# A chunked linear recurrence with routed layers: the order of VectorE's work over four chunks, and the engine that masks the grams

## The chip, the cores and the metric

One NeuronCore of a Trainium2 chip runs the whole program. The metric is the device time of one execution in microseconds (us), lower is better. Engines are named as in the profile: PE is TensorE, DVE VectorE, ACT ScalarE, POOL GpSimd, SP the engine that only issues transfers.

## What is computed

Inputs r, k, v, w, a, b are (4 batches, 8 heads, 768 steps, 40 channels), all float32. Each of the 32 pairs of batch and head runs a recurrence over a 40x40 state:

```python
for t in range(768):
    y[:, :, t] = np.einsum('bhd,bhde->bhe', rt, state)
    Sa = np.einsum('bhde,bhe->bhd', state, at)
    state = state * wt[:, :, None, :] - np.einsum('bhd,bhe->bhde', Sa, bt)
    state = state + np.einsum('bhd,bhe->bhde', vt, kt)
```

y goes, as 3072 tokens of 320 values, through a layer of 8 experts (the best two of noisy gates, 320 to 1024 to 320, relu) and a dense layer (320 to 2048 to 320, leaky relu). The change touches the recurrence alone.

## The kernel before

Four stages follow one another: `stage_a` is the recurrence, `stage_r` the routing, `stage_e` the experts, `stage_m` the dense layer. Only `stage_a` matters here. It lays the recurrence out in 24 chunks of 32 steps, indexed `k`; four chunks make a group `s` of 128 steps (`s = k // 4`, place in the group `c = k % 4`, `NS_` = 6 groups, `NK` = 24 chunks). The state (`S0T`) is handed from chunk to chunk. For each group there are products that don't need the state, made ahead of time:

- `suffix(s)` (DVE) turns the loaded decays `P` into running products, `prefix(s)` (DVE) does so for `U`. `make_A`, `make_B`, `make_K` (POOL) multiply the loaded `AT` with `U` and `BT`, `KT` with `P`.
- The grams: `lb(s, c)` (PE, from `AT` and `BT`) gives the coupling of the steps inside a chunk; ACT copies it to `LbS`, SP writes it to DRAM (`out_half`), reads it back by lanes (`to_lanes`, tile `Lt`), and DVE inverts it there by substitution: `inverse(s)` is a generator of 63 steps, first the clearing of `Tl` (after a wait for `Lt` and for the write of the last `Tl`), then for t = 1 to 31 a product `prod` of t x t elements (L331) and a reduction (L335). The result goes to DRAM and back as blocks (`from_lanes`, `to_blocks`, tile `TT`, 16 transfers), for `solve` on PE.
- `lk(s, c)` (from `KT` and `AT`) goes to `LkT`, `gv(k)` to `GvT`, `gp(k)` to `Gpb`. ACT copies each out of PSUM, and each is then multiplied in place by a triangular mask `pos_m` or `neg_m`: `mask_lk`, `mask_gv`, `mask_gp`.

PE runs a hand-written order: in chunk k it does `first(k)` (L532), a gram of a later group, `turn_S(k)` (L596), `grow_K`, `solve(k)` (L606), `read_S(k-1)`, `add_B(k-1)` (L648, needs the masked `Gpb` of k-1), `turn_P`, `gv`, `grow_B`, tokens or rows, a second gram, `add_K(k-1)` (L658, needs the masked `GvT` of k-1), `gp(k)` (L665), and `lkv(k+1)` (L542, needs the masked `LkT`). `turn_S(k)` writes the banks in which the outputs of chunk k-2 lie, so it waits until DVE has read them: `pe.wait_ge(q["v_y"], k - 1)`, that is, until `y_out(k-2)` (L355) is done. `first(k)` at c = 0 waits for `decay(s-1)` (L344), which scales the state by `Wend`.

SP's queue is in order too. At c = 2 and 3 it issues `out_half(s+2, c-2)`, which waits for ACT's copies of the grams `lb`; at c = 3 there follow, in this order:

```python
                if c >= 2 and s + 2 < NS_:
                    out_half(s + 2, c - 2)
                if c == 3 and s + 1 < NS_:
                    from_lanes(s + 1)
                    if s + 2 < NS_:
                        to_lanes(s + 2)
                    to_blocks(s + 1)
                    if s + 3 < NS_:
                        suffix_in(s + 3)
```

`from_lanes(s+1)` waits for the end of `inverse(s+1)`; `suffix_in(s+3)` is the load of `P`. At the next c = 0 the loads of `AT`, `BT`, `KT` follow, and at c = 1 that of `U`, which waits for `v_y` of 4s, the last output of the group before. `zeros` are loads into `xsort` that nothing here waits for; ACT issues `RV` and `Vd` for chunk k+2 at the end of each chunk.

DVE takes, in each chunk, `y_out(k-2)` and then a number of steps of `inverse(s+1)`: 14, 12, 18 and the 19 that are left, with `suffix(s+2)` after eight steps at c = 0 and `prefix(s+2)` after eleven at c = 1; `decay` comes at the start of the next group.

Of the kernel before, what the change touches and what calls it, by code (L numbers as in the profile page):

```python
# [21 lines left out]
ALU = mybir.AluOpType  # L22
# [5 lines left out]
CH = 32  # L28
NS_ = S // SC
NK = S // CH  # L30
# [12 lines left out]
def stage_a(nc, st, wE, wR, aE, bE, kE, rvE, vG, cst, wgh, zer, lscr, tscr, xrow, xsort):  # L43
    ctx = ExitStack()
    with ctx:
# [3 lines left out]
        def sem(name):  # L49
# [4 lines left out]
        pos_m = sb("pos_m", [128, CH])  # L54
        neg_m = sb("neg_m", [128, 128])
# [12 lines left out]
        LkT = sb("LkT", [128, 2, 4, 2, 4, CH])  # L68
# [16 lines left out]
                 "l_lw l_lane l_tw l_t0 l_t1 l_t2 l_t3 l_zf l_x0 l_x1 "  # L85
                 "z_v z_g e_A e_B e_K v_P v_U v_end v_dve v_inv v_y v_S "
                 "o_S o_X o_y p_X p_Gv p_G p_Str p_P p_tok p_rows p_PT p_S p_y p_Gp "
                 "a_X a_gv a_G a_S0 a_Pn a_tok a_row a_PT a_S a_Gp g_lk g_gv g_gp").split()
        q = {n: sem(n) for n in names}
        block = ctx.enter_context(nc.Block())  # L90
        TOKS = {0: (0,), 1: (), 2: (1, 2), 3: (3,)}
# [1 line left out]
        def slot(k):  # L93
            return k // 4, k % 4
# [11 lines left out]
        def round_lk(s, c):  # L106
            return 4 + c if s == 0 else before(4 * (s - 1) + c // 2) + c % 2
# [113 lines left out]
        def _(pool):  # L221
# [20 lines left out]
                    i = tt(t, t, P[:, :, CH * c:CH * c + CH].rearrange("p (b h) t -> p h b t", b=NB), ALU.mult)  # L242
                i.then_inc(q["e_K"], 1)

            def mask_lk(s, c):
                pool.wait_ge(q["a_G"], round_lk(s, c) + 1)
                t = LkT[:, s % 2, c, :, :, :].rearrange("p h g t -> p (h g) t")
                tt(t, t, pos_m[:, :].rearrange("p (o t) -> p o t", o=1).to_broadcast([128, 8, CH]), ALU.mult).then_inc(q["g_lk"], 1)

            def mask_gv(k):  # L250
                pool.wait_ge(q["a_gv"], k + 1)
                t = GvT[:, k % 2, :, :, :].rearrange("p h b t -> p (h b) t")
                tt(t, t, pos_m[:, :].rearrange("p (o t) -> p o t", o=1).to_broadcast([128, 8, CH]), ALU.mult).then_inc(q["g_gv"], 1)

            def mask_gp(k):
                pool.wait_ge(q["a_Gp"], k + 1)
                t = Gpb[:, :, :, :].rearrange("p b h m -> p (b h) m")
                tt(t, t, neg_m[:, :].rearrange("p (o t) -> p o t", o=1).to_broadcast([128, 8, 128]), ALU.mult).then_inc(q["g_gp"], 1)

            make_A(0, 0)  # L260
            make_A(0, 1)
            make_K(0)
            pool.wait_ge(q["l_c"], 80)
            for c in range(4):
                mask_lk(0, c)
            for j in range(2):
                make_A(1, j)
                make_B(1, j)
            make_K(1)
            for k in range(NK):  # L270
                s, c = slot(k)
                mask_gv(k)
                if c < 2 and s + 1 < NS_:
                    mask_lk(s + 1, 2 * c)
                    mask_lk(s + 1, 2 * c + 1)
                if c == 1 and s + 2 < NS_:
                    for j in range(2):
                        make_A(s + 2, j)
                        make_B(s + 2, j)
                if c == 2 and s + 2 < NS_:  # L280
                    make_K(s + 2)
                mask_gp(k)

        @block.vector
        def _(dve):
# [63 lines left out]
            def y_out(k):  # L349
                s, c = slot(k)  # L350
                dve.wait_ge(q["p_y"], k + 1)
                if k and c == 0:
# [3 lines left out]
                                        ps[0:EP, 2:4, 0:256].rearrange("p i (g t) -> p i g t", t=CH),  # L356
                                        U[:, s % 3, :, t].rearrange("p (i g) t -> p i g t", i=2), ALU.mult).then_inc(q["v_y"], 1)

            nc.vector.memset(ps[:, :, :], 0.0).then_inc(q["z_v"], 1)
            nc.vector.memset(start[:, :], 0.0).then_inc(q["z_v"], 1)  # L360
            dve.wait_ge(q["z_v"], 2)
# [14 lines left out]
            prefix(1)  # L376
            for _ in T:
                pass
            steps = {0: 14, 1: 12, 2: 18, 3: 64}
            for k in range(NK + 2):  # L380
                s, c = slot(k)
                if k < NK and c == 0:
                    T = inverse(s + 1) if s + 1 < NS_ else iter(())
                    if k:
                        decay(s - 1)
                if k >= 2:
                    y_out(k - 2)
                if k >= NK:
                    continue
                for i in range(steps[c]):  # L390
                    if c == 0 and i == 8 and s + 2 < NS_:
                        suffix(s + 2)
                    if c == 1 and i == 11 and s + 2 < NS_:
                        prefix(s + 2)
                    next(T, None)

        @block.scalar
        def _(act):
# [121 lines left out]
        def _(pe):  # L520
# [15 lines left out]
            def lkv(k):  # L536
                s, c = slot(k)
                pe.wait_ge(q[f"l_g{k % 2}"], 16 * (k // 2 + 1))
                pe.wait_ge(q["g_lk"], 4 * s + c + 1)
                for p in range(2):  # L540
                    for h in range(4):
                        m = mm(ps[Z_[h], 4 + p, 0:NB * D], LkT[:, s % 2, c, p, h, :], Vd[:, k % 2, p, h, :],  # L542
                               start=True, stop=False, skip_group_check=True)
                m.then_inc(q["o_X"], 1)
# [146 lines left out]
            for k in range(NK + 1):  # L691
# [29 lines left out]
                if k:  # L721
                    if k < NK:
                        pe.wait_ge(q["a_S0"], k + 1)
                    else:
                        pe.wait_ge(q["v_y"], k - 1)
                    read_S(k - 1, 0)
                    pe.wait_ge(q["g_gp"], k)
                    add_B(k - 1)
                if k < NK:
                    pe.wait_ge(q["a_PT"], k + 1)  # L730
# [15 lines left out]
                if k:  # L746
                    pe.wait_ge(q["o_y"], 4 * k - 3)
                    read_S(k - 1, 1)
                    pe.wait_ge(q["g_gv"], k)
                    pe.wait_ge(q["o_y"], 4 * k - 1)  # L750
                    add_K(k - 1, 0)
                if k < NK:
# [691 lines left out]
```

## Time and profile before

| | us |
|---|---|
| median of 3 runs | 1638.34 (1636.05 to 1650.76) |
| the profiled execution's own time | 1636.78 |
| its span | 1635.0 |
| busy in the span: PE, DVE, ACT, POOL | 1341.4, 909.5, 655.1, 304.8 |

The time of an execution is that of its span and 1.8 us around it. The span's first 642 us are the recurrence; in rows of the profile, a time such as 275.39 is counted from the start of the span, "idle before" is how long the engine had nothing running, and the name behind the arrow is what ended that. Busy shares over the whole span say little about the recurrence, since the later stages have other limits.

### The profile page before, as it was taken

What the parts mean: (1) busy time and instruction counts of PE and PEld (TensorE: products, weight loads), DVE (VectorE), ACT (ScalarE), POOL (GpSimd) and SP (SyncE); (2) the same over time, 40 slices, a digit from 0 to 9 for tenths busy, and PEclk for the clock granted to TensorE, in tenths of its full rate; (3) what the DMA queues carried; (4) which work ended last, traced back from release to release, by engine and by line L of the source; (5) the groups of instructions that cost most, each with busy time, mean ns of one, the idle gap of its engine ahead of it and who ended that gap; (6) DMA issues with size and microseconds to landing.
All of it is one profiled execution on the core that took longest, in us unless ns stands there. A gap on an engine that the chain in (4) does not pass through costs nothing. (4 is left out here: it accounts for less than half of the span.)

```text
span 1635.0 us, 40604 instructions
## 1 busy us (share of the span) xinstructions
PE 1341.4 (82%) x16814; PEld 1217.7 (74%) x16814; DVE 909.5 (56%) x1553; ACT 655.1 (40%) x1451; POOL 304.8 (19%) x253
## 2 busy tenths in 40 slices
PE   3549698888979796004999999999993999999998
PEld 3437586666868585004999999999993889889887
DVE  4857557492663401504777777778772453554533
ACT  3314334343434122203666666666661333333332
POOL 3316132241411110570000000000003210110000
PEclk9957767686687665556999999999997999999999
DMA  6753554748352222735676676676661110110000
GB/s 153 176 112 100 126 157 119 202 119 193 113 145 81 76 71 64 266 120 172 216 259 216 218 255 218 219 253 218 222 214 53 53 32 17 49 38 10 16 17 16
DMA packets 149248, 219.58 MB, mean 134 GB/s; under 512 B 61210, under 2 KB 120474, under 8 KB 145722
## 3 DMA queue, kind: packets, MB, share of 16 engines
q1 hardware_dynamic: 132143, 163.84, 34.4%
q10 hardware_dynamic: 9891, 27.97, 5.8%
q0 software_dynamic: 7088, 25.89, 4.8%
q8 instruction: 103, 1.69, 0.4%
q14 instruction: 23, 0.19, 0.0%
HBM read 185.49 MB, written 42.34 MB: 139 GB/s over the span
## 5 line engine op out<-in xcount | busy, mean ns | idle before, releaser
L1232 DVE TENSOR_TENSOR gf<-psM,low 128x512 f32<-128x512 f32 x96 | 66.4, 692 | 179.3 <-ACT low L1270 179.3
L331 DVE TENSOR_TENSOR prod<-Tl,Lt 128x1 f32<-128x1 f32 (+30 forms) x186 | 142.9, 768 | 38.0 <-DMA Lt<-lscr 31.9
L1075 PE MATMUL psE<-w2h,hh 128*128 128x320 f32 x496 | 155.9, 314 | 0.0
L1270 ACT ACTIVATE low<-psM 128x512 f32<-128x512 f32 x96 | 57.5, 599 | 242.6 <-PE psM L1328 242.6
L1077 PE MATMUL psE<-w2h,hl 128*128 128x320 f32 x496 | 153.5, 309 | 0.0
L1076 PE MATMUL psE<-w2l,hh 128*128 128x320 f32 x496 | 153.4, 309 | 0.0
L1060 PE MATMUL psE<-xh,w1h 128*128 128x256 f32 x496 | 141.6, 285 | 5.6 <-DVE w1l L965 5.6
L1061 PE MATMUL psE<-xl,w1h 128*128 128x256 f32 x496 | 141.5, 285 | 0.0
L1062 PE MATMUL psE<-xh,w1l 128*128 128x256 f32 x496 | 141.5, 285 | 0.0
L965 DVE TENSOR_TENSOR w2l<-w2t,w2h 128x320 fp32r<-128x320 f32 x248 | 122.1, 492 | 10.8 <-ACT w2h L960 10.8
L1307 PE MATMUL psM<-woh,gh 128*128 128x320 f32 x384 | 120.1, 313 | 2.9 <-DVE gl L965 2.5
L1132 DVE SCALAR_TENSOR_TENSOR hl<-psE,hh 128x256 fp32r<-128x256 f32 x248 | 105.4, 425 | 27.6 <-ACT hh L1101 4.3
L1309 PE MATMUL psM<-woh,gl 128*128 128x320 f32 x384 | 118.8, 309 | 0.0
L1308 PE MATMUL psM<-wol,gh 128*128 128x320 f32 x384 | 118.7, 309 | 0.0
L1101 ACT ACTIVATE hh<-psE 128x256 fp32r<-128x256 f32 x248 | 95.0, 383 | 55.2 <-PE psE L1064 52.9
L960 ACT ACTIVATE w2h<-w2t 128x320 fp32r<-128x320 f32 x248 | 114.8, 463 | 0.0
L1147 POOL DMA_DIRECT2D ysort<-ys x31 | 22.2, 717 | 483.8 <-DVE ys L1139 483.8
L965 DVE TENSOR_TENSOR w1l<-w1t,w1h 128x1024 fp32r<-128x1024 f32 (+1 forms) x93 | 108.1, 1218 | 2.1
L1042 PE MATMUL psE<-ident,xs 128*128 128x128 f32 x186 | 26.1, 278 | 92.2 <-DMA w1t<-in_w_dram 92.2
L1060 PEld LDWEIGHTS psE<-xh,w1h 128*128 128x128 f32 x496 | 96.3, 194 | 6.0 <-issue 6.0
L335 DVE TENSOR_REDUCE Tl<-prod 128x1 f32<-128x1 f32 (+30 forms) x186 | 93.7, 504 | 5.9
L355 DVE TENSOR_TENSOR xT<-psA,U 104x512 f32<-104x512 f32 x24 | 16.5, 689 | 144.2 <-PE psA L658 144.2
(170 smaller groups left out, 3378.9 us busy)
## 6 DMA issues: line engine op xcount, KB each, us to landing
w2t<-in_w_dram SPq DMA_DIRECT2D x31, 1280.0 KB, 6.2
w1t<-in_w_dram SPq DMA_DIRECT2D x31, 1024.0 KB, 8.1
w1t<-in_w_dram SPq DMA_DIRECT2D x62, 256.0 KB, 8.8
Vd<-in_vG_dram ACTq DMA_DIRECT2D x22, 640.0 KB, 6.2
xs<-xsort SPq DMA_DIRECT2D x31, 320.0 KB, 5.7
ysort<-ys POOLq DMA_DIRECT2D x31, 320.0 KB, 4.3
xsort<-in_zer_dram SPq DMA_DIRECT2D x15, 640.0 KB, 8.3
RV<-in_rvE_dram ACTq DMA_DIRECT2D x22, 416.0 KB
```

The source lines that it names most:

```text
L331: mark(nc.vector.tensor_tensor(prod[:, 0:t, 0:t], Tl[:, 0:t, CH - t:CH], Lt[:, t:t + 1, CH - t:CH].to_broadcast([128, t, t]), ALU.mult))
L960: return nc.scalar.activation(hi, src, ACT.Copy)
L965: return nc.vector.tensor_tensor(lo, src, hi.bitcast(F32), ALU.subtract)
L1060: mm(o, w1h[:, j, fs], xh[:, p, j, :], start=(j == 0), stop=False)
L1061: mm(o, w1h[:, j, fs], xl[:, p, j, :], start=False, stop=False)
L1062: mm(o, w1l[:, j, fs], xh[:, p, j, :], start=False, stop=False)
L1075: mm(o, hh[:, f, sl], w2h[:, f, :], start=(f == 0), stop=False)
L1076: mm(o, hh[:, f, sl], w2l[:, f, :], start=False, stop=False)
L1077: m = mm(o, hl[:, f, sl], w2h[:, f, :], start=False, stop=(f == NF - 1))
L1307: mm(o, gh[:, f % 4, sl], woh[:, f, :], start=(f == 0), stop=False)
L1308: mm(o, gh[:, f % 4, sl], wol[:, f, :], start=False, stop=False)
L1309: m = mm(o, gl[:, f % 4, sl], woh[:, f, :], start=False, stop=(f == NF - 1))
```

## The change

On POOL `mask_lk` stays for group 0 alone, the other masks go, and `make_B`, `make_K`, `make_A` get a new order. On DVE the masks are added, each waiting for ACT's copy, and the steps of the inversion, `suffix`, `prefix` and `decay` get new places: 10 + 17 steps at c = 0 behind `suffix`, 10 + 8 at c = 1, 6 + 6 at c = 2, 6 at c = 3, with `decay(s)` at the end of c = 3. PE's order is as it was; only the names of what it waits for change. SP and ACT are untouched.

```diff
--- before.py
+++ after.py
@@ -85,7 +85,7 @@
                  "l_lw l_lane l_tw l_t0 l_t1 l_t2 l_t3 l_zf l_x0 l_x1 "
                  "z_v z_g e_A e_B e_K v_P v_U v_end v_dve v_inv v_y v_S "
                  "o_S o_X o_y p_X p_Gv p_G p_Str p_P p_tok p_rows p_PT p_S p_y p_Gp "
-                 "a_X a_gv a_G a_S0 a_Pn a_tok a_row a_PT a_S a_Gp g_lk g_gv g_gp").split()
+                 "a_X a_gv a_G a_S0 a_Pn a_tok a_row a_PT a_S a_Gp g_lk v_lk v_gv v_gp").split()
         q = {n: sem(n) for n in names}
         block = ctx.enter_context(nc.Block())
         TOKS = {0: (0,), 1: (), 2: (1, 2), 3: (3,)}
@@ -242,44 +242,30 @@
                     i = tt(t, t, P[:, :, CH * c:CH * c + CH].rearrange("p (b h) t -> p h b t", b=NB), ALU.mult)
                 i.then_inc(q["e_K"], 1)
 
-            def mask_lk(s, c):
-                pool.wait_ge(q["a_G"], round_lk(s, c) + 1)
-                t = LkT[:, s % 2, c, :, :, :].rearrange("p h g t -> p (h g) t")
+            def mask_lk(c):
+                pool.wait_ge(q["a_G"], round_lk(0, c) + 1)
+                t = LkT[:, 0, c, :, :, :].rearrange("p h g t -> p (h g) t")
                 tt(t, t, pos_m[:, :].rearrange("p (o t) -> p o t", o=1).to_broadcast([128, 8, CH]), ALU.mult).then_inc(q["g_lk"], 1)
-
-            def mask_gv(k):
-                pool.wait_ge(q["a_gv"], k + 1)
-                t = GvT[:, k % 2, :, :, :].rearrange("p h b t -> p (h b) t")
-                tt(t, t, pos_m[:, :].rearrange("p (o t) -> p o t", o=1).to_broadcast([128, 8, CH]), ALU.mult).then_inc(q["g_gv"], 1)
-
-            def mask_gp(k):
-                pool.wait_ge(q["a_Gp"], k + 1)
-                t = Gpb[:, :, :, :].rearrange("p b h m -> p (b h) m")
-                tt(t, t, neg_m[:, :].rearrange("p (o t) -> p o t", o=1).to_broadcast([128, 8, 128]), ALU.mult).then_inc(q["g_gp"], 1)
 
             make_A(0, 0)
             make_A(0, 1)
             make_K(0)
             pool.wait_ge(q["l_c"], 80)
             for c in range(4):
-                mask_lk(0, c)
+                mask_lk(c)
             for j in range(2):
                 make_A(1, j)
                 make_B(1, j)
             make_K(1)
             for k in range(NK):
                 s, c = slot(k)
-                mask_gv(k)
-                if c < 2 and s + 1 < NS_:
-                    mask_lk(s + 1, 2 * c)
-                    mask_lk(s + 1, 2 * c + 1)
+                if c == 0 and s + 2 < NS_:
+                    make_B(s + 2, 0)
+                    make_B(s + 2, 1)
                 if c == 1 and s + 2 < NS_:
-                    for j in range(2):
-                        make_A(s + 2, j)
-                        make_B(s + 2, j)
-                if c == 2 and s + 2 < NS_:
                     make_K(s + 2)
-                mask_gp(k)
+                    make_A(s + 2, 0)
+                    make_A(s + 2, 1)
 
         @block.vector
         def _(dve):
@@ -356,6 +342,24 @@
                                         ps[0:EP, 2:4, 0:256].rearrange("p i (g t) -> p i g t", t=CH),
                                         U[:, s % 3, :, t].rearrange("p (i g) t -> p i g t", i=2), ALU.mult).then_inc(q["v_y"], 1)
 
+            def tiled(m, n):
+                return m.rearrange("p (o t) -> p o t", o=1).to_broadcast([128, 8, n])
+
+            def mask_lk(s, c):
+                dve.wait_ge(q["a_G"], round_lk(s, c) + 1)
+                t = LkT[:, s % 2, c, :, :, :].rearrange("p h g t -> p (h g) t")
+                nc.vector.tensor_tensor(t, t, tiled(pos_m[:, :], CH), ALU.mult).then_inc(q["v_lk"], 1)
+
+            def mask_gv(k):
+                dve.wait_ge(q["a_gv"], k + 1)
+                t = GvT[:, k % 2, :, :, :].rearrange("p h b t -> p (h b) t")
+                nc.vector.tensor_tensor(t, t, tiled(pos_m[:, :], CH), ALU.mult).then_inc(q["v_gv"], 1)
+
+            def mask_gp(k):
+                dve.wait_ge(q["a_Gp"], k + 1)
+                t = Gpb[:, :, :, :].rearrange("p b h m -> p (b h) m")
+                nc.vector.tensor_tensor(t, t, tiled(neg_m[:, :], 128), ALU.mult).then_inc(q["v_gp"], 1)
+
             nc.vector.memset(ps[:, :, :], 0.0).then_inc(q["z_v"], 1)
             nc.vector.memset(start[:, :], 0.0).then_inc(q["z_v"], 1)
             dve.wait_ge(q["z_v"], 2)
@@ -376,23 +380,51 @@
             prefix(1)
             for _ in T:
                 pass
-            steps = {0: 14, 1: 12, 2: 18, 3: 64}
+            dve.wait_ge(q["l_c"], 80)
             for k in range(NK + 2):
                 s, c = slot(k)
+
+                def invert(n):
+                    for _ in range(n):
+                        next(T, None)
+
                 if k < NK and c == 0:
                     T = inverse(s + 1) if s + 1 < NS_ else iter(())
-                    if k:
-                        decay(s - 1)
                 if k >= 2:
                     y_out(k - 2)
+                if 1 <= k <= NK:
+                    mask_gp(k - 1)
                 if k >= NK:
                     continue
-                for i in range(steps[c]):
-                    if c == 0 and i == 8 and s + 2 < NS_:
+                if c == 0:
+                    if s + 2 < NS_:
                         suffix(s + 2)
-                    if c == 1 and i == 11 and s + 2 < NS_:
+                    invert(10)
+                    mask_gv(k)
+                    if s + 1 < NS_:
+                        mask_lk(s + 1, 0)
+                    invert(17)
+                    if s + 1 < NS_:
+                        mask_lk(s + 1, 1)
+                elif c == 1:
+                    invert(10)
+                    mask_gv(k)
+                    if s + 1 < NS_:
+                        mask_lk(s + 1, 2)
+                    if s + 2 < NS_:
                         prefix(s + 2)
-                    next(T, None)
+                    invert(8)
+                    if s + 1 < NS_:
+                        mask_lk(s + 1, 3)
+                elif c == 2:
+                    invert(6)
+                    mask_gv(k)
+                    invert(6)
+                else:
+                    invert(6)
+                    mask_gv(k)
+                    if s + 1 < NS_:
+                        decay(s)
 
         @block.scalar
         def _(act):
@@ -536,7 +568,7 @@
             def lkv(k):
                 s, c = slot(k)
                 pe.wait_ge(q[f"l_g{k % 2}"], 16 * (k // 2 + 1))
-                pe.wait_ge(q["g_lk"], 4 * s + c + 1)
+                pe.wait_ge(q["v_lk" if s else "g_lk"], 4 * (s - 1 if s else 0) + c + 1)
                 for p in range(2):
                     for h in range(4):
                         m = mm(ps[Z_[h], 4 + p, 0:NB * D], LkT[:, s % 2, c, p, h, :], Vd[:, k % 2, p, h, :],
@@ -724,7 +756,7 @@
                     else:
                         pe.wait_ge(q["v_y"], k - 1)
                     read_S(k - 1, 0)
-                    pe.wait_ge(q["g_gp"], k)
+                    pe.wait_ge(q["v_gp"], k)
                     add_B(k - 1)
                 if k < NK:
                     pe.wait_ge(q["a_PT"], k + 1)
@@ -746,7 +778,7 @@
                 if k:
                     pe.wait_ge(q["o_y"], 4 * k - 3)
                     read_S(k - 1, 1)
-                    pe.wait_ge(q["g_gv"], k)
+                    pe.wait_ge(q["v_gv"], k)
                     pe.wait_ge(q["o_y"], 4 * k - 1)
                     add_K(k - 1, 0)
                 if k < NK:
```

## Rows read from the trace of the kernel before

**Rows 1.** Windows by chunk (4, 5, 16): length, busy by engine, PEclk, DMA share, GB/s.

```profile
179.60:199.20 19.60, 18.74 (x459) 14.66 (x461) 2.65 (x10) 8.28 (x20) 2.68 (x4) 0.76 0.68 130
199.20:235.40 36.20, 28.59 (x492) 24.92 (x492) 16.79 (x36) 9.81 (x28) 9.30 (x7) 0.59 0.69 180
...
466.10:485.70 19.60, 18.72 (x456) 14.62 (x457) 4.84 (x19) 8.28 (x20) 2.54 (x4) 0.76 0.72 160
```

**Rows 2.** Waits, 0 to 650 us: who <- whom, us in total, times, longest.

```profile
PE psA L606 <- DMA TT<-tscr: 23.0, 2, 20.0
PE psA L532 <- DVE S0T L344: 22.7, 5, 5.6
...
PE psA L596 <- DVE xT L355: 5.6, 2, 3.2
```

**Rows 3.** PE's timeline, chunks 7 to 11: start, duration, engine, line, [idle before <-releaser].

```profile
253.28 0.77 PE L532 MATMUL psA<-S0T,AT 40*32 40x40 f32 x64 [0.18 <-PE psA L542]
...
275.39 0.94 PE L532 MATMUL psA<-S0T,AT 40*32 40x40 f32 x64 [4.57 <-DVE S0T L344]
...
303.39 1.65 PE L596 MATMUL psA<-ident,S0T 104*128 104x104 f32 x8 [3.16 <-DVE xT L355]
...
328.92 0.93 PE L532 MATMUL psA<-S0T,AT 40*32 40x40 f32 x64 [0.18 <-PE psA L542]
...
346.10 0.77 PE L532 MATMUL psA<-S0T,AT 40*32 40x40 f32 x64 [0.18 <-PE psA L542]
```

**Rows 4.** Timeline of SP and DVE from the end of chunk 7.

```profile
266.81 0.35 SPq L147 DMA_DIRECT2D lscr<-LbS  x1
...
274.64 0.32 SPq L161 DMA_DIRECT2D tscr<-Tl  x1
...
291.06 0.58 SPq L132 DMA_DIRECT2D xsort<-in_zer_dram  x1
...
294.79 0.06 DVE L299 MEMSET start<- 104x4 f32 x1 [11.66 <-DMA P<-in_wR_dram]
...
302.65 0.68 DVE L355 TENSOR_TENSOR xT<-psA,U 104x512 f32<-104x512 f32 x1
```

**Rows 5.** Instructions by line, 0 to 600 us.

```profile
L242 POOL TENSOR_TENSOR KT<-KT,P 104x512 f32<-104x512 f32 x24 | 31.5, 1345 | 0.2 <-DMA KT<-in_kE_dram 0.2
...
L367 DVE TENSOR_TENSOR BT<-BT,P 104x1024 f32<-104x1024 f32 x2 | 2.3, 1210 | 0.0
```

**Rows 6.** Waits of SP's queue, 0 to 640 us.

```profile
SPq L155 <- DMA lscr<-LbS: 3.2, 1, 3.2
```

**Rows 7.** DVE's small steps, t = 1 and t = 7.

```profile
472.58 0.16 DVE L331 TENSOR_TENSOR prod<-Tl,Lt 128x1 f32<-128x1 f32 x1 [2.75 <-DMA Lt<-lscr]
...
475.07 0.21 DVE L331 TENSOR_TENSOR prod<-Tl,Lt 128x49 f32<-128x49 f32 x1
```

**Rows 8.** DVE beside POOL at chunk 17.

```profile
485.30 2.34 POOL L258 TENSOR_TENSOR Gpb<-Gpb,neg_m 128x1024 f32<-128x1024 f32 x1 [1.56 <-ACT Gpb L402]
485.50 2.23 DVE L331 TENSOR_TENSOR prod<-Tl,Lt 128x64 f32<-128x64 f32 x1
...
490.48 0.34 DVE L331 TENSOR_TENSOR prod<-Tl,Lt 128x169 f32<-128x169 f32 x1
```

**Rows 9.** The transfer that SP issued at 291.06: size, us to landing.

```profile
xsort<-in_zer_dram SPq DMA_DIRECT2D x1, 640.0 KB, 23.0
```

**Rows 10.** DVE and POOL at chunk 2.

```profile
139.74 2.19 POOL L235 TENSOR_TENSOR BT<-BT,P 104x1024 f32<-104x1024 f32 x1
...
140.69 3.60 DVE L331 TENSOR_TENSOR prod<-Tl,Lt 128x196 f32<-128x196 f32 x1
...
141.88 2.20 POOL L229 TENSOR_TENSOR AT<-AT,U 104x1024 f32<-104x1024 f32 x1
```

**Rows 11.** Chunks 0 to 1.

```profile
114.66 0.06 DVE L299 MEMSET start<- 104x4 f32 x1 [10.56 <-DMA P<-in_wR_dram]
...
127.11 1.07 PE L648 MATMUL psA<-Gpb,Bk 128*40 128x128 f32 x16
```

## The prediction

> **What bounds the kernel now.** I read the page's row of busy shares by slice, then windows by chunk, then who waited for whom, then the timelines around the longest waits. Only the first 642 us of the span can change. There PE is the engine that work passes through: it is busy 18.7 of the 19.6 us of chunk 4, but only 28.6 of the 36.2 us of chunk 5, at a mean granted clock of 0.76 and 0.59 [rows 1], so part of its time is waiting and part is the half clock around the waits. The waits by name are three [rows 2]: for the scaled state at the start of a group (22.7 us in five times), for `y_out` of the last chunk of the old group at `turn_S` of chunk 4s+1 (5.6 us, two times), and for the inverse's blocks (23.0 us, of which 20.0 at the very start and 3.0 in group 5). Behind them stands a loop over three queues. I measure a group from the start of its predecessor's chunk c = 3, here chunk 7 at 253.28 [rows 3]:
>
> - SP passes `out_half` at 266.81, which is 13.5 us in, when ACT has copied the last gram; the inverse, which is DVE's long tail of 19 steps, ends just before SP's next issue at 274.64; `P` lands at 294.79, 20.15 us after that (21.8 and 22.1 us in the two other groups of this kind) [rows 4].
> - DVE, which stood idle 11.66 us for `P`, does `suffix`, six small steps and `y_out` by 303.33, 8.5 us later (7.0 and 6.9 in the two other groups, where no POOL instruction fell on the scans) [rows 4]. PE's `turn_S(9)` starts at 303.39 after a wait of 3.16 us [rows 3].
> - From there PE takes 25.5 us to the start of chunk 10 and 17.2 more to chunk 11 [rows 3], where the loop closes.
>
> So `turn_S(9)` starts 50.1 us behind the start of chunk 7 (49.3 and 49.2 in the two other groups), and this number, not the sum of DVE's work, decides the recurrence's pace.
>
> **The change: what it gives.** `decay(s)` follows in chunk c = 3 behind six steps and `mask_gv`. Six steps are at most six instructions of 1.21 us, the duration of a product of 1024 elements [rows 5], 7.3 us; with `y_out` (0.68 [rows 4]) and `mask_gp` (1.2, by the same row of 1024 elements) DVE is through after 9.2 us of a chunk in which PE has 16 us of work. The waits at `first` go: 22.7 us. The inverse then ends at most 9.2 us into chunk 7, not 21.4. But SP can't use that: `out_half(s+2, 1)` stands ahead of `from_lanes` in its queue and passes 13.5 us in [rows 4]. Of 12 us that the inverse gains, 7.9 reach the queue. Of these, 2.5 go again: `to_lanes` waits for the write of `LbS`, which had 7.8 us of lead and now is issued right ahead; the bounds are 0 and the 3.2 us that such a wait once took [rows 6]. A further 2.0 go since ACT's loads `RV` and `Vd` (1.08 MB by their shapes) leave at the end of chunk 7 and now meet the small block transfers; bounds 0 and 6.7, all of it at 160 GB/s [rows 1]. With 21.3 as the mean from the issue to the landing, `P` lands 13.5 + 2.5 + 21.3 + 2.0 = 39.3 us into the count (34 to 45), where it was 41.5: a gain of 2.2.
>
> The masks leave POOL, where nothing but DVE felt them; PE waited once for one, 1.3 us at the end, which goes.
>
> **What it costs.** `y_out(4s-1)` now stands behind all of c = 0: `suffix`, 27 steps and three masks, and PE's `turn_S(4s+1)` is who waits. From the landing of `P`:
>
> - what was there before: 7.0;
> - the clearing of `Tl`, 1.0 (1024 elements, estimate by the 1.21 of [rows 5]), and seven first steps that used to be done while `P` was on its way: 13 steps from t = 1 to the product of t = 7 take 2.7 us [rows 7], so 1.4;
> - 13 more steps, to t = 13: from the product of t = 8 to that of t = 13 are 5.3 us, of which 2.0 are blocking (next item) [rows 8]; with the two reductions at the ends 3.9;
> - three masks of 256 elements: a quarter of 1.21, 1.0 in all.
>
> That is 14.3 us. To it comes the blocking. A product of 64 elements beside POOL's mask took 2.23 us and ended with it [rows 8], where one of 169 took 0.34. In the new order POOL starts `make_B` twice and `make_K` right behind `suffix`, as soon as `BT` and `KT` are there. These follow `P` in SP's queue. The last transfer of that series lands at 291.06 + 23.0 = 314.06 [rows 4, 9]; `AT`, `BT`, `KT` (832 KB each by shape) and its own 640 KB moved in the 17.9 us since 296.2, when the `zeros` ahead of them was in by the same view, so `BT` is there some 11 us and `KT` some 16 us behind `P` (an estimate by bytes). Two `make_B` of 2.2 us [rows 10] then fall on the small steps, each holding up one product: 3.5. Of four `make_K` instructions of 1.35 us [rows 5] the last one or two products and the last mask meet up to three: between 0 and 3.6, and I take 1.2, since most of the steps are done by then. Sum 19.0 us (14.3 to 21.5), against 7.0 to 8.5.
>
> How long one product is held has a rule beside it. In chunk 2 a product of 196 elements started at 140.69 while POOL's `BT` ran until 141.93, and it ended 3.60 us later, after the next POOL instruction too [rows 10]. The Trainium skill, "SBUF — State Buffer", section "SBUF: two separate sides", says that the port pair VectorE and GpSimd share is a lock, held for a whole instruction by whichever starts first. By that rule a waiting product would lose one POOL instruction at most; by the row it can lose two. By the row, both `make_B` may fall on one product, and the steps behind it start some 0.5 us later than by the rule, 19.5 in place of 19.0.
>
> So `turn_S` of c = 1 starts 39.3 + 19.0 = 58.3 us into the count: 8.2, 9.0 and 9.1 us later than before in groups 1, 2 and 3 taken together, 26.3. PE's wait there becomes some 18 us (its own work reaches `turn_S` 16 + 22.7 us in), and takes the place of both old waits. It adds nothing elsewhere: `prefix` waits for `U`, issued with `y_out(4s-1)`, but chunk c = 1 is the long one, 25.5 us behind `turn_S` [rows 3]. The masks' own waits cover themselves: `mask_gv` waits for a copy in mid-chunk, and behind it at c = 2 stand six steps of under 1.2 us each, which fit ahead of the chunk's end.
>
> In group 0 there is no `y_out` to wait for, but `mask_gp(0)` stands behind the same list. `P` is there at 114.66 [rows 11], no `zeros` are ahead of `BT`, so all of `make_K` falls on the steps: 114.66 + 14.3 - 0.7 + 3.5 + 3.0 + 1.2 = 136.0, while `add_B(0)` started at 127.11 [rows 11]. PE waits 8.8 us (2.3 to 10). `y_out(0)` at chunk 2 then comes late by 2.7 more (0 to 5), behind `prefix` and 18 steps. Together 11.5.
>
> After the last `suffix`, in groups 4 and 5, the change only gives: the wait at chunk 16 (5.4 of the 22.7), at chunk 20 (1.7), that for the blocks (3.0), the mask (1.3), and the half clock behind the two waits. Chunk 16 ran at 0.76 [rows 1]; a quarter of its 19.6 us is lost to the clock and I give back 3.0, and 2.0 in chunk 20. Sum 16.4. The four other waits at `first` are inside the counts above. For a shorter c = 1, with the loads behind it and fewer gaps in PE's fetching, I take off 1.0 each, 3.0.
>
> **Sum.** 26.3 + 11.5 - 16.4 - 3.0 = +18.4 us. The profiled execution took 1636.8 us; it becomes 1655.2. It lies 1.6 below the median shown, so in terms of the median it is about 1656.
>
> **Rivals.** *The wait moves and costs nothing.* POOL's instructions find DVE idle, or `KT` lands late, and the small steps run unblocked: 14.3 in place of 19.0, and group 0 loses 3 in place of 11.5. Then 12.2 + 3 - 16.4 - 3.0 = -4, 1633 to 1645 around it. For it: the product of t = 13 and its neighbours are short, 0.3 us [rows 8], and rarely meet anything. Against: [rows 8] shows that even 64 elements wait.
>
> *Faster: the chain from the inverse to `P` shortens.* Its 16 block transfers ran beside the first chunk's loads; started 8 us sooner they may take less, with neither the 2.5 nor the 2.0 paid. The point from which it decides is `turn_S` at 49.5 us into the count. At 13.5 + 18 + 14.3 = 45.8 each group gains 3.7, in all -11 + 3 - 16.4 - 3.0 = -27, about 1610. For it: the gain at `first` is certain. Against: it needs all three terms at their low ends.
>
> *Slower still.* All terms at their high ends, 45 + 21.5 = 66.5 us: 17 more a group, 1680. Chunk 5 was at 0.59 of the full clock already [rows 1], so little is left to lose there.
>
> **How the numbers follow.** The sum as worked out (1646 to 1672) 0.5; the unblocked case 0.28; the faster one 0.13; the heavier one 0.09. A measurement of this kernel tells changes of over 1%, 16.4 us, from none, so the bounds are 1622 and 1655. Above 1655 lie half of the first case, part of the space between, and the last: 0.45. Below 1622 lies the faster case with an edge of the second: 0.15. Within 0.40. The range 1618 to 1672 leaves out the faster case and the heavier one.
>
> **What would show it.** Right: PE's wait at L532 for S0T gone; a wait of PE at L596 for DVE xT of 12 to 20 us in each of groups 1 to 3; at L648 for DVE Gpb of some 9 us in chunk 1; SP's `tscr` issue right behind the `lscr` issue, 13 to 14 us into c = 3; DVE idle for `P` over 20 us; products at t = 8 to 13 of over 1.3 us. Wrong: L596 waits of under 8 us, small steps without blocking, or `P` landing less than 34 us into the count.

## The result and the profile after

The changed kernel takes 1660.4 us (median of 4 runs, 1658.4 to 1666.8), the kernel before 1641.6 (4 runs). The medians lie 18.8 us apart; the ratio is 1.013, with a 95% interval of 1.009 to 1.017, so the loss is 14 to 28 us. The forecast was 1656. The execution that was profiled took 1666.8 us, the longest of the four, so its rows show some 6 us more than the median has, while the profile of the kernel before (1636.8) is 5 us below its own median. The two profiles lie 30.0 us apart, and some 11 us of that is the spread of executions.

The waits by name, 0 to 680 us (who <- whom, us in total, times, longest). In the changed file L564 is `first`, L628 `turn_S`, L638 `solve`, L680 `add_B`, L285 the start of `suffix`, L341 `y_out`:

```profile
DVE start L285 <- DMA P<-in_wR_dram: 87.9, 5, 24.3
...
PE psA L628 <- DVE xT L341: 34.5, 4, 11.4
...
PE psA L638 <- DMA TT<-tscr: 33.0, 5, 19.5
...
PE psA L680 <- DVE Gpb L361: 9.0, 2, 8.6
```

Beside [rows 2]: the wait at `first` for the scaled state (22.7 us) has left the list. The one at `turn_S` for `y_out` has grown from 5.6 to 34.5, the one at `solve` for blocks from 23.0 to 33.0, and `add_B`, which waited 1.3 us for a mask once, now waits 8.6 us for one in chunk 1.

The same stretch as in [rows 3, 4], chunks 7 to 10, on PE, then SP and DVE:

```profile
273.67 0.77 PE L564 MATMUL psA<-S0T,AT 40*32 40x40 f32 x64 [0.18 <-PE psA L574]
...
291.50 0.93 PE L564 MATMUL psA<-S0T,AT 40*32 40x40 f32 x64 [0.18 <-PE psA L574]
...
311.64 0.63 PE L564 MATMUL psA<-S0T,AT 40*32 40x40 f32 x49 [0.18 <-PE psA L574]
...
328.87 1.65 PE L628 MATMUL psA<-ident,S0T 104*128 104x104 f32 x8 [9.39 <-DVE xT L341]
...
355.57 0.93 PE L564 MATMUL psA<-S0T,AT 40*32 40x40 f32 x64 [0.18 <-PE psA L574]
```

```profile
280.20 1.16 DVE L321 TENSOR_REDUCE Tl<-prod 128x31 f32<-128x961 f32 x1
...
287.31 0.35 SPq L147 DMA_DIRECT2D lscr<-LbS  x1
287.84 0.32 SPq L161 DMA_DIRECT2D tscr<-Tl  x1
...
306.26 1.42 SPq L127 DMA_DIRECT2D P<-in_wR_dram  x1
...
314.29 0.06 DVE L285 MEMSET start<- 104x4 f32 x1 [22.30 <-DMA P<-in_wR_dram]
...
328.13 0.69 DVE L341 TENSOR_TENSOR xT<-psA,U 104x512 f32<-104x512 f32 x1
```

Read from the start of chunk 7 (273.67): SP passes the gram's write 13.6 us in and issues the inverse right behind it, although DVE had ended it at 281.36, 6.5 us before that issue (5.9, 11.9 and 7.2 us in chunks 3, 11 and 15); `P` lands 40.6 us in; `y_out` ends after 55.2 us, and `turn_S(9)` starts with it. Before, those were 13.5, 41.5 and 50.1. Chunk 8 starts without a wait at its head, 17.8 us in, where it was 22.1.

Windows of chunks 4, 5 and 16, columns as in [rows 1]:

```profile
187.30:213.30 26.00, 21.78 (x458) 16.98 (x460) 1.65 (x3) 8.29 (x20) 0.00 (x0) 0.70 0.78 153
213.30:255.30 42.00, 26.78 (x492) 23.20 (x493) 38.47 (x69) 9.81 (x28) 15.07 (x8) 0.58 0.50 135
495.80:521.20 25.40, 18.02 (x456) 14.05 (x457) 10.17 (x34) 8.29 (x20) 0.00 (x0) 0.83 0.83 178
```

DVE is nearly idle in chunk 4 (1.65 us of 26.0) and full in chunk 5 (38.5 of 42.0): its work was not spread. Chunk 16 grew from 19.6 to 25.4 us; PE waits 6.4 us in it for blocks, at `solve`.

DVE and POOL behind `P`'s landing in group 1, at 212.11 (start, duration):

```profile
222.50 4.31 POOL L235 TENSOR_TENSOR BT<-BT,P 104x1024 f32<-104x1024 f32 x2 [71.25 <-DMA BT<-in_bE_dram]
222.54 2.23 DVE L317 TENSOR_TENSOR prod<-Tl,Lt 128x81 f32<-128x81 f32 x1
...
225.08 1.84 DVE L317 TENSOR_TENSOR prod<-Tl,Lt 128x100 f32<-128x100 f32 x1
...
227.96 5.98 POOL L242 TENSOR_TENSOR KT<-KT,P 104x512 f32<-104x512 f32 x4 [1.16 <-DMA KT<-in_kE_dram]
```

`BT` is there 10.4 us behind `P`, `KT` 15.9 us (estimated: 11 and 16). Each `make_B` held up one product, t = 9 by 2.0 and t = 10 by 1.6 us. In group 2 SP had issued one more of the `zeros` ahead of these loads, and `BT` came only 16.3 us behind `P`, after `y_out`: no step was held there. In group 3 it came 12.2 us behind `P`.

### The profile page after: what moved, and what is told of

It is laid out like the page before. It is cut to its first block and busy times, and to the rows that moved or that the text cites. A ratio compares the mean times of both kernels' runs of the same rounds, so it can differ in the third digit from the quotient of the medians.

```text
span 1665.1 us, 40604 instructions
## 1 busy us (share of the span) xinstructions
PE 1349.9 (81%) x16814; PEld 1221.4 (73%) x16814; DVE 940.4 (56%) x1621; ACT 655.8 (39%) x1451; POOL 213.6 (13%) x185
## 3 DMA queue, kind: packets, MB, share of 16 engines
q8 instruction: 103, 1.69, 0.4%
## 5 line engine op out<-in xcount | busy, mean ns | idle before, releaser
L317 DVE TENSOR_TENSOR prod<-Tl,Lt 128x1 f32<-128x1 f32 (+30 forms) x186 | 130.2, 700 | 29.4 <-DMA Lt<-lscr 23.6
L1164 DVE SCALAR_TENSOR_TENSOR hl<-psE,hh 128x256 fp32r<-128x256 f32 x248 | 105.4, 425 | 27.6 <-ACT hh L1133 4.4
L1094 PEld LDWEIGHTS psE<-xh,w1l 128*128 128x128 f32 x496 | 96.2, 194 | 0.0
L1093 PEld LDWEIGHTS psE<-xl,w1h 128*128 128x128 f32 x496 | 96.1, 194 | 0.0
```

The lines of the kernel that those rows point to most:

```text
L317: mark(nc.vector.tensor_tensor(prod[:, 0:t, 0:t], Tl[:, 0:t, CH - t:CH], Lt[:, t:t + 1, CH - t:CH].to_broadcast([128, t, t]), ALU.mult))
L1093: mm(o, w1h[:, j, fs], xl[:, p, j, :], start=False, stop=False)
L1094: mm(o, w1l[:, j, fs], xh[:, p, j, :], start=False, stop=False)
```

## The experiments

Each kernel is compared with the kernel before, run on the same chip in turn, whose median was 1642.8, 1642.2 and 1640.5 us in the three rounds; "ratio" is its time over that. The changed kernel's 1.013 comes from a round of its own, with four executions on each side.

**One part at a time.** The masks alone, the same three helpers defined on DVE (`mask_lk` of group 0 stays on POOL):

```diff
             for k in range(NK):
                 s, c = slot(k)
-                mask_gv(k)
-                if c < 2 and s + 1 < NS_:
-                    mask_lk(s + 1, 2 * c)
-                    mask_lk(s + 1, 2 * c + 1)
...
-                mask_gp(k)
...
                 if k >= 2:
                     y_out(k - 2)
+                if 1 <= k <= NK:
+                    mask_gp(k - 1)
...
                     next(T, None)
+                mask_gv(k)
+                if c < 2 and s + 1 < NS_:
+                    mask_lk(s + 1, 2 * c)
+                    mask_lk(s + 1, 2 * c + 1)
```

> The order of before on DVE (14, 12, 18 and 19 steps, decay at the start of the next group) and on POOL for make_A, make_B, make_K; only the masks are moved to DVE, mask_gp behind y_out, mask_gv and mask_lk at the end of a chunk's steps. Theory (the time went into y_out of the last chunk of a group, which stands behind all of c = 0): the masks add 1.6 us a chunk to DVE, of which some 2 us stand ahead of decay in c = 3, and take away blocking by POOL of 1 to 2 us there; 0 to 3 us a group, 1638 to 1652 us, and the wait at turn_S of c = 1 stays under 5 us. Rival (the masks themselves cost it, by DVE's work and its waits for ACT): most of the 20 us, 1655 or more.

1641.3 us, ratio 0.999 (0.996 to 1.002). The waits of its profile:

```profile
PE psA L620 <- DMA TT<-tscr: 24.2, 6, 18.4
...
PE psA L546 <- DVE S0T L329: 10.5, 4, 4.6
PE psA L610 <- DVE xT L340: 10.3, 3, 5.4
...
PE psA L576 <- POOL BT L235: 4.3, 1, 4.3
```

The masks cost nothing; the wait for the scaled state (L546) even halves, while the one at `turn_S` (L610) doubles. The rival that blames the masks by themselves is out.

The order alone:

```diff
+                if c == 1 and s + 2 < NS_:
+                    make_K(s + 2)
                 mask_gv(k)
...
                 if c == 1 and s + 2 < NS_:
-                    for j in range(2):
-                        make_A(s + 2, j)
-                        make_B(s + 2, j)
-                if c == 2 and s + 2 < NS_:
-                    make_K(s + 2)
+                    make_A(s + 2, 0)
+                    make_A(s + 2, 1)
                 mask_gp(k)
+                if c == 0 and s + 2 < NS_:
+                    make_B(s + 2, 0)
+                    make_B(s + 2, 1)
...
-                    if k:
-                        decay(s - 1)
...
-                for i in range(steps[c]):
-                    if c == 0 and i == 8 and s + 2 < NS_:
-                        suffix(s + 2)
-                    if c == 1 and i == 11 and s + 2 < NS_:
+                if c == 0 and s + 2 < NS_:
+                    suffix(s + 2)
+                for i in range((27, 18, 12, 6)[c]):
+                    if c == 1 and i == 10 and s + 2 < NS_:
                         prefix(s + 2)
                     next(T, None)
+                if c == 3 and s + 1 < NS_:
+                    decay(s)
```

> The new order of steps, suffix, prefix and decay on DVE, but all masks stay on POOL, with mask_gp of c = 0 ahead of make_B and the masks of c = 1 behind make_K. Theory: turn_S of c = 1 waits as in the changed kernel, less 1 us for the masks that are gone, 8 to 11 us in groups 1 to 3; the wait of add_B(0) for the mask (8.6 us) goes; 1646 to 1655 us. Rival (the masks cost it): the waits go with the masks, 1620 to 1640 us.

1671.1 us, ratio 1.016 (1.011 to 1.021). The order alone (on DVE and on POOL) loses at least as much as the whole change. My range ended 16 us too low, since I had thought that it would be a little cheaper than the whole change. Its waits at `turn_S` are 42.3 us in four, 12.6 at most. From `P` to `turn_S` it takes 20.3, 17.6 and 19.1 us in groups 1 to 3, where the changed kernel takes 19.3, 14.6 and 17.7. In groups 2 and 3 POOL's `mask_gp` falls beside DVE's scans of `P`, which take 6.64 us in place of 4.61. In group 2:

```profile
316.80 2.35 POOL L258 TENSOR_TENSOR Gpb<-Gpb,neg_m 128x1024 f32<-128x1024 f32 x1 [2.24 <-ACT Gpb L403]
316.87 0.06 DVE L301 MEMSET start<- 104x4 f32 x1 [23.64 <-DMA P<-in_wR_dram]
316.96 6.64 DVE L306 TENSOR_TENSOR_SCAN P<-P,start 104x516 f32<-104x516 f32 x4
```

So here the masks on POOL do cost something that they don't cost on DVE. Whether that is the whole of the difference was not tried.

**The blocking.** The changed kernel with `make_A`, `make_B` in turn behind `prefix` and `make_K` at c = 2:

```diff
-                if c == 0 and s + 2 < NS_:
-                    make_B(s + 2, 0)
-                    make_B(s + 2, 1)
                 if c == 1 and s + 2 < NS_:
-                    make_K(s + 2)
-                    make_A(s + 2, 0)
-                    make_A(s + 2, 1)
+                    for j in range(2):
+                        make_A(s + 2, j)
+                        make_B(s + 2, j)
+                if c == 2 and s + 2 < NS_:
+                    make_K(s + 2)
```

> The changed kernel with make_B and make_K of POOL back in their old places (A, B, A, B behind prefix, K at c = 2), so that no POOL instruction falls on the small steps of c = 0. Theory with blocking: from P's landing to y_out it takes 14.3 us in place of 14.6 to 19.3, the wait of add_B(0) falls from 8.6 to 2.5 us; PE has to wait a little for BT at c = 2; 1643 to 1652 us. Rival (blocking doesn't matter, the steps are hidden): 1658 to 1663 us.

1653.4 us, ratio 1.007 (1.003 to 1.011). From `P`'s landing to the end of `y_out`, in group 1:

```profile
208.65 0.06 DVE L284 MEMSET start<- 104x4 f32 x1 [25.06 <-DMA P<-in_wR_dram]
...
222.50 0.69 DVE L340 TENSOR_TENSOR xT<-psA,U 104x512 f32<-104x512 f32 x1
```

14.5 us where the sum for unblocked steps was 14.3, and 19.3 in the changed kernel. It takes 14.5 us in groups 2 and 3 too. The wait of `add_B(0)` is 3.5 in place of 8.6 us, and one of 2.6 us for `BT` is new in chunk 2. So the blocking is real and is gone. What it is worth in the whole is less sure: 7.0 us of 18.8 by the medians, 0.6 of 1.3 points by the ratios, whose intervals overlap. The waits at `turn_S` fell only from 34.5 to 31.8 us in total, as PE came to them earlier.

**`y_out` out of the way of `P`.** The changed kernel with `suffix` in c = 1:

```diff
                 if c == 0:
-                    if s + 2 < NS_:
-                        suffix(s + 2)
                     invert(10)
...
                 elif c == 1:
+                    if s + 2 < NS_:
+                        suffix(s + 2)
                     invert(10)
```

> The changed kernel with suffix(s+2) moved from the start of c = 0 to c = 1, behind y_out and mask_gp, so that y_out of the old group's last chunk waits for no load. Theory: the waits of turn_S in c = 1 (9.4 to 11.4 us, three) and of add_B(0) (8.6 us) go; the loop then closes over the load of U and make_A at c = 2, where PE waits up to 7 us a group; 1610 to 1635 us. Rival (the masks cost it): no gain, 1655 us or more.

1642.7 us, ratio 1.001 (0.998 to 1.004). The loss is gone, as the theory says and the rival (no gain, 1655 us or more) does not; but the 1610 to 1635 I had expected was not reached. Waits:

```profile
PE psA L638 <- DMA TT<-tscr: 28.2, 5, 18.8
...
PE psA L564 <- issue: 9.4, 3, 4.3
PE psA L671 <- issue: 7.4, 4, 3.4
PE psA L628 <- DVE xT L341: 7.4, 2, 3.8
```

At `turn_S` 7.4 us are left of 34.5. The wait for `make_A` at c = 2 that I had expected did not come. What stays is the blocks at `solve` (28.2 with the 18.8 of the very start, so 9.4 where the kernel before had 3.0), and what came forward is "issue", time in which PE waited for nothing that the profile shows. PE's sum of "issue" over 76 to 642 us is 29.2 us in the kernel before, 28.2 in the changed one and 37.4 here.

**SP's queue.** The next four kernels change where SP issues. The loads of `P` ahead of `out_half`:

```diff
+                if c == 3 and s + 3 < NS_:
+                    suffix_in(s + 3)
                 if c == 0 and s + 2 < NS_:
...
                     to_blocks(s + 1)
-                    if s + 3 < NS_:
-                        suffix_in(s + 3)
```

> The changed kernel, but SP issues the load of P for suffix(s+3) at the start of c = 3, ahead of out_half, instead of behind the block transfers. Theory (what costs is the wait for P, 22 to 24 us of idle VectorE, with y_out behind it): P is there when c = 0 begins, the waits of turn_S in c = 1 of groups 1 to 3 (9.4 to 11.4 us) fall under 3 us, and what remains late is the blocks at solve in c = 0, 2 to 6 us a group; group 0 is unchanged; 1625 to 1645 us. Rival (the order on VectorE is simply too long for the chunk, whatever the load does): the waits stay over 7 us, 1655 or more.

1650.2 us, ratio 1.006 (1.004 to 1.009). The waits of `turn_S(4s+1)` are gone in all three groups, and DVE no longer waits for `P` there. What stays is group 0 (9.1 us at `add_B`), blocks at 1.9 to 3.0 us a group, and 36.5 us of "issue". So the waits behind `P` are gone, and half of the loss stayed; 5 us slower than expected.

The blocks ahead:

```diff
+                if c == 3 and s + 1 < NS_:
+                    from_lanes(s + 1)
+                    to_blocks(s + 1)
                 if c >= 2 and s + 2 < NS_:
                     out_half(s + 2, c - 2)
                 if c == 3 and s + 1 < NS_:
-                    from_lanes(s + 1)
                     if s + 2 < NS_:
                         to_lanes(s + 2)
-                    to_blocks(s + 1)
```

> The changed kernel, but SP issues from_lanes and to_blocks at c = 3 ahead of out_half(s+2, 1), to_lanes behind it. Theory: the inverse that ends 9 us into c = 3 now reaches SP; the waits of solve for blocks at c = 0 (2.8, 1.6, 2.7, 6.4 us) go. In groups 1 to 3 nothing comes of it unless P lands earlier too, since turn_S waits later in the same stretch; P stands behind to_lanes, whose gate is as before, but the 16 block transfers (8 us) are no longer ahead of it, so P lands up to 8 us earlier: 1625 to 1650 us. Rival (the blocks' transfers cost the same wherever they stand, P does not come earlier): 1650 to 1660 us.

1647.8 us, ratio 1.004 (1.000 to 1.007). Two lines of its waits:

```profile
PE psA L629 <- DVE xT L342: 31.4, 4, 12.1
...
PE psA L639 <- DMA TT<-tscr: 19.7, 1, 19.7
```

Only the very first wait for blocks is left, the other four (2.8, 1.6, 2.7 and 6.4 us) are gone, with the gate of `out_half` passed by: SP issues the inverse 7.7 us into chunk 3, where it was 13.6. This shows that the inverse, ready early, was held in SP's queue. `P` lands 36.9, 36.6 and 35.8 us into the count, 4 to 10 us earlier, yet `turn_S` waits only 3 us less in all, since PE too comes to it earlier.

Both:

> The changed kernel with both edits of SP's order: P ahead, and blocks ahead of out_half. Theory: only PE's own work, fetching and the half clock are left in c = 0 and c = 1; groups of 84 to 90 us against 98 in the changed kernel and 94 before; 1595 to 1625 us. Rival: no better than the better one of the two alone.

1631.0 us, ratio 0.996 (0.992 to 0.999). Better than either alone, but far from 1595 to 1625. Neither `y_out` nor blocks are late in groups 1 to 5; "issue" is 44.4 us.

With `suffix(2)` behind `mask_gp(0)` in group 0 as well:

```diff
                 if c == 0:
-                    if s + 2 < NS_:
+                    if s and s + 2 < NS_:
                         suffix(s + 2)
                     invert(10)
...
                 elif c == 1:
+                    if s == 0:
+                        suffix(2)
                     invert(10)
```

> The kernel with both edits of SP's order, and for group 0 alone suffix(2) moved from c = 0 to c = 1, behind mask_gp(0). Theory (add_B(0) waits for a mask that stands behind the load of P): the wait of 9.1 us in chunk 1 goes, that of 3.8 us at turn_S of chunk 2 grows by at most 3, so 6 to 9 us less than with both edits alone: 1620 to 1627 us. Rival (the clear time comes back in chunk 2 in full): as with both edits, 1631 us.

1628.7 us, ratio 0.992 (0.989 to 0.995), 12 us under the kernel before by the medians of that round: the version that beats both. `add_B(0)` doesn't wait. PE's longest waits in chunks 1 to 23:

```profile
PE psA L674 <- issue: 11.2, 6, 4.2
PE psA L631 <- DVE xT L342: 8.2, 2, 4.4
PE psA L641 <- issue: 7.7, 2, 4.3
PE psA L567 <- issue: 7.1, 2, 3.6
PE psA L655 <- issue: 7.0, 4, 4.3
```

45.6 us of "issue" in all. One is in the middle of `read_S`, chunk 4, where the matmuls before and behind it are of the same kind and no semaphore stands between them:

```profile
200.24 0.27 PE L655 MATMUL psA<-RV,S 40*40 40x32 f32 x7
204.81 0.63 PE L655 MATMUL psA<-RV,S 40*40 40x32 f32 x25 [4.30 <-issue]
```

**The gain alone.** The kernel before with a shorter tail and `decay(s)` in c = 3:

```diff
-            steps = {0: 14, 1: 12, 2: 18, 3: 64}
+            steps = {0: 14, 1: 20, 2: 18, 3: 11}
...
-                    if k:
-                        decay(s - 1)
...
+                if c == 3 and s + 1 < NS_:
+                    decay(s)
```

> The kernel before with one part of the change: 14, 20, 18 and 11 steps in place of 14, 12, 18 and 19, and decay(s) at the end of c = 3; suffix stays behind eight steps of c = 0, the masks stay on GpSimd, and GpSimd's order is the old one. Theory: the waits at first for the scaled state (22.7 us in five) go, y_out of c = 1 still waits only for P and six steps, 0 to 5 us; the blocks now come late at solve by 1 to 3 us as in the changed kernel; 1620 to 1635 us. Rival (a wait removed at the start of a group comes back elsewhere in full): 1636 to 1645 us.

1648.1 us, ratio 1.004 (1.001 to 1.007): my theory for it fell. The rival (the wait comes back elsewhere in full, 1636 to 1645 us) is nearer, and the time is even 3 us above it. The wait at `first` is gone, and this stands in its place:

```profile
PE psA L606 <- DMA TT<-tscr: 26.3, 5, 18.5
...
PE psA L596 <- DVE xT L355: 18.4, 6, 5.8
```

Six waits at `turn_S`, the two longest at c = 2 (5.8 us in chunks 6 and 10), where the eight steps that I had put behind `prefix` at c = 1 now stand ahead of `y_out`. It does not price `decay` alone, since my edit made a wait of its own.

**The loads of RV and Vd.** The changed kernel with those of c = 3 held back:

```diff
                 copy(GvT[:, k % 2, :, :, :].rearrange("p h b t -> p (h b t)"), ps[:, 4, 256:512], "a_gv")
+                if k and c == 0:
+                    chunk(k + 1)
...
-                if k + 2 < NK:
+                if k + 2 < NK and c != 3:
                     chunk(k + 2)
```

> The changed kernel, but ACT's loads of RV and Vd at the end of c = 3 wait until the copy of GvT in the next chunk, some 13 us, so that they don't meet the transfers between the inverse's end and P. Theory (these loads and the gate of LbS made the blocks late at solve of c = 0): SP issues the blocks within 6 us of the inverse's, where it took 9 to 11, the waits at solve (2.8, 1.6, 2.7, 6.4 us) fall under 1.5 us, P lands 2 to 5 us earlier, but chunk 5, 9 and 13 may wait for Vd; 1648 to 1658 us. Rival (the transfers of the inverse are slow by themselves): unchanged, 1660.

1653.8 us, ratio 1.009 (1.006 to 1.012). SP in the changed kernel (first fence, at chunk 15 to 16) and in this one (second, chunk 3 to 4):

```profile
493.85 0.32 SPq L161 DMA_DIRECT2D tscr<-Tl  x1
495.40 8.03 SPq L155 DMA_DIRECT2D Lt<-lscr  x4
503.53 9.36 SPq L171 DMA_DIRECT2D TT<-tscr  x16
```

```profile
184.93 0.32 SPq L161 DMA_DIRECT2D tscr<-Tl  x1
186.51 3.47 SPq L155 DMA_DIRECT2D Lt<-lscr  x4
190.50 8.86 SPq L171 DMA_DIRECT2D TT<-tscr  x16
...
207.87 0.06 DVE L285 MEMSET start<- 104x4 f32 x1 [19.03 <-DMA P<-in_wR_dram]
```

The issue of the four `Lt` reads takes 3.5 us in place of 8.0, the blocks follow 5.6 us behind the inverse in place of 9.7, and `P` lands 36.9, 34.9 and 34.6 us into the count in place of 41.3, 40.6 and 45.8. Counted from the issue of the inverse, `P` lands after 22.9, 20.6 and 20.9 us in place of 27.6, 26.5 and 26.2: 4.7 to 5.8 us sooner. The rest of the third (45.8) is `out_half`, which passed 19.1 us in there and 13.2 here. No `solve` waits for blocks after the first. The theory of the loads is right. But PE waits 13.3, 8.7, 6.6 and 1.9 us at `lkv`. The profile calls that "issue"; by its place it is the wait for the held-back `Vd`, and it takes most of the gain back: 1653.8 us is not clear of the changed kernel's 1660.4.

All together:

> Both edits of SP's order, suffix(2) behind mask_gp(0), and ACT's later loads, together. If each gives what it gives alone: 1612 to 1624 us. Rival (PE is now bound by its own work and by fetching behind the loads, which are only moved): as the best of the others, 1625 us.

1641.7 us, ratio 1.001 (0.998 to 1.004): a miss. The later loads cost 13 us beside the best version, 14.5 us of "issue" at `lkv` and 59.1 in all.

## Why the prediction was right

The direction, the place and the size were as forecast: +18.4 us, and the medians lie 18.8 apart. That they agree to half a microsecond is luck: the two profiles are 30.0 apart, and several terms were off and made up for one another. Point by point:

- *The wait for the scaled state goes.* So it was. It gives up its 22.7 us, and none came back at `first`.
- *SP holds the inverse back.* Right: `out_half` passed 13.1, 13.6 and 19.1 us into c = 3 and the inverse was issued 0.5 us behind it; with the blocks ahead of that gate, four waits vanished.
- *P lands 39.3 us into the count.* 41.3, 40.6 and 45.8. Of the two terms of it, the wait of `to_lanes` was set too high, at 2.5: between the inverse's issue and the first `Lt` read there are 1.1 to 1.4 us. The meeting with `RV` and `Vd` was set too low, at 2.0: it is worth 4.7 to 5.8 us by the run that takes it away. The third landing is late because chunk 11 itself was longer, 23.2 us, and `out_half` passed late in it.
- *From P to y_out 19.0 us.* 19.3, 14.6 and 17.7 to the start of `turn_S`; unblocked 14.5 for the 14.3 summed. `BT` and `KT` came as estimated in group 1 alone. In group 2 `BT` came 16.3 us behind `P` and nothing was held: the rival in which the steps run unblocked is what happened there. So two products in each group is an upper case.
- *How long one product is held.* The Trainium skill, "SBUF — State Buffer", section "SBUF: two separate sides", calls the shared port pair an exclusive lock that is held for a whole instruction. Read so, a product loses one GpSimd instruction at most. In the rows of the changed kernel shown above each did. In other runs it did not: beside the 3.60 us of [rows 10], a product took 3.98 us in the run of the order alone (t = 20, 0.6 us unheld) and 3.60, 4.06, 4.07 and 4.01 us in the run of the gain alone, each time until just behind POOL's second instruction of some 2.2 us. So the row, and not the rule, is the bound.
- *`turn_S` starts 58.3 us into the count.* 60.6, 55.2 and 63.5, 59.8 on average: `P` 3.3 us later than summed and the steps behind it 1.8 us shorter, the latter because group 2 had no blocking. PE's waits there are 11.4, 9.4 and 9.9, not 18, and below the 12 to 20 that I had named as a sign: chunks 4, 8 and 12 took 26.0, 20.1 and 27.4 us, for they were now late by blocks and "issue". Late work hid behind later work. Products of over 1.3 us, another sign, are there in groups 0, 1 and 3 and not in group 2.
- *Group 0.* 8.6 and 3.8 us for 8.8 and 2.7.
- *Up to chunk 16* the sum was +29.4 us (26.3 + 11.5 - 5.4 - 3.0), and the profile has chunk 16 start 29.7 us later (495.8 against 466.1). Two errors cancel in it: `turn_S` was 30.7 us later in all and not 26.3, and from it to the next c = 3 PE took 7.8 us less in all, where I had taken off 3.0.
- *Groups 4 and 5.* Here a term failed. I gave back 11 us: 5.0 for the clock, 3.0 for blocks, 1.7 and 1.3 for waits. From the start of chunk 16 to the start of the next stage it is 179.3 us, before 179.1. Chunk 16 lost 5.8 us to the blocks, which I had held to be in time; its granted clock rose from 0.76 to 0.83, which is worth 0.6 us at most (25.4 less the wait of 6.4 is 19.0, against 19.6). Chunk 20 gave its 5.8 us, but chunks 17 to 19 gave none. The run with the blocks ahead of `out_half` bears this out: with no wait for blocks the same stretch takes 170.6 us, 8.5 less than before. In the profiled execution the sum is 11.6 us too low, in the medians 4; how much of the 11.6 is this term and how much the spread of executions can't be told from one profile of each.
- *Small slips.* 1655.2 and 1.6 are 1656.8. The three delays of `turn_S` belong to groups 2, 1 and 3 in this order. Neither changes anything. No run prices the 1.0 us a group that I took off for fewer gaps in PE's fetching; "issue" was 29.2 us before and 28.2 in the changed kernel.

## What to carry to other kernels

When steps are moved on an in-order engine, ask which instruction with a foreign waiter now stands behind a load, and count from the load's landing to that instruction; the busy share of the engine says nothing of it. A result that is ready earlier is worth only what the queue that must issue it lets through: look for the gate ahead of it (the inverse lay ready for 5.9 to 11.9 us here), and for the large transfers that it now meets. And when a wait is taken away at the head of a stage, check what was hidden behind it, since here each wait removed brought out the next: the state, then `y_out`, then blocks, then PE's own gaps.

## What was not expected of the hardware

- PE stands up to 5.6 us in the middle of a run of equal matmuls, with no releaser in the profile. "Issue" in all is 28.2 us in the changed kernel and 45.6 us in the fastest one, in which PE waits least for others. The gaps inside a run stand at the same place of PE's program in different kernels: in `first(9)` ahead of the last 15 of the 64 matmuls, 2.05 us in the kernel before, 4.81 in the changed one, 3.60 in the fastest, and between 1.8 and 4.8 us in eleven of the thirteen kernels. In six such gaps, of these three kernels, one packet of the profile's "instruction" DMA queue falls 2.1 to 3.1 us ahead of the gap's end; this queue moves 103 packets and 1.69 MB in a whole execution, 16 KB each. That points to PE waiting for its own instructions, behind the bulk loads. It was not tried by a run that moves only this, and it does not hold for all of "issue": the 13.3 us at `lkv` above are most likely a load.
- From the changed kernel to the fastest one, PE's waits fell by 26.3 us at `turn_S`, 14.0 at `solve` and 8.6 at `add_B`, 48.9 in all. "Issue" rose by 17.4, and the median fell by 31.7.
- Four reads of 128 KB took 8.0 us to issue while `RV` and `Vd` were on their way, and 3.5 us without them. It need not be the reads: in chunk 8 they took 3.1 us and the 16 block reads behind them 13.5, in place of 9.3. From the inverse's issue to that of `P` there are 18.4 to 19.3 us with the meeting, 13.9 to 14.6 without. So a queue that only issues can itself be slowed by another queue's transfers.
